# Attention, soft MoE and switch MoE in one kernel: block sums of values moved beside a pair's first scores, their copy moved to ScalarE, exponentials signalled singly

## The reference

```python
# q, k, v: (4 batches, 8 heads, 768, 64); nb = 24 blocks of 32 keys
k_sum = k.reshape(B, H, nb, block, D).max(axis=3)
v_sum = v.reshape(B, H, nb, block, D).mean(axis=3)
mask_l = np.abs(pos[:, None] - pos[None, :]) < window      # window = 16
scores_l = scale * q @ k.T
scores_s = scale * q @ k_sum.T + np.log(block)
a = softmax(concat([where(mask_l, scores_l, -1e9), scores_s]))
x = a @ concat([v, v_sum])
```

## Time and profile before

| | us |
|---|---|
| median of 3 runs (lowest, highest) | 379.94 (379.44, 381.62) |
| the profiled execution, device time | 379.92 |
| its span, first to last instruction | 378.2 |
| PE, DVE, ACT, POOL busy over the span | 326.6, 175.9, 143.6, 101.1 |
| attention stage, to the last weighted values | about 122.5 |
| granted TensorE clock, mean over the span | 0.969 of full speed |

### The profile page before, as it was taken

How to read it: one execution, slowest core, us unless ns; L and a number is a source line. 1 busy time by engine, 2 the same in 40 slices (tenths; PEclk the granted TensorE clock), 3 DMA queues, 4 the chain that set the end, 5 groups by cost and what they waited for, 6 DMA issues and landing times.

```text
span 378.2 us, 9016 instructions
## 1 busy us (share of the span) xinstructions
PE 326.6 (86%) x3272; PEld 233.9 (62%) x3273; DVE 175.9 (47%) x406; ACT 143.6 (38%) x329; POOL 101.1 (27%) x181
## 2 busy tenths in 40 slices
PE   0879879889898999969877795999999999999991
PEld 0556656667677754232325264788888888888880
DVE  2577867877885553360116596132331323213231
ACT  1476666666876422310110262123232322313221
POOL 5665675676764000000000000121211212112121
PEclk9999999999999999987998999699999999999996
DMA  7999999999999716999942900110101111010110
GB/s 306 362 425 408 414 423 415 419 419 420 410 385 406 297 50 227 383 390 405 393 156 83 364 2 0 57 47 36 55 28 55 41 42 55 28 55 34 49 56 32
DMA packets 23851, 81.64 MB, mean 216 GB/s; under 512 B 2312, under 2 KB 2312, under 8 KB 21776
## 3 DMA queue, kind: packets, MB, share of 16 engines
q1 hardware_dynamic: 20640, 73.08, 49.1%
q0 software_dynamic: 1920, 6.29, 4.4%
q10 hardware_dynamic: 1264, 1.92, 1.5%
HBM read 74.99 MB, written 6.29 MB: 215 GB/s over the span
## 4 chain that ended last, share of the span: by engine, by line
PE 57%; DMA 16%; DVE 11%; ACT 4%; POOL 4%; issue 4%; SPq 2%; ACTq 0%; DVEq 0%; POOLq 0%
PE ps L904 33%; DMA ring<-in_vt 11%; DMA ring<-in_moe_w 5%; PE ps L630 3%; POOL ring L503 3%; PE ps L643 3%; PE ps L890 3%; PE ps L600 3%; ACT work L962 2%; PE ps L787 2%; SPq L285 2%; PE ps L746 2%; DVE ps L1128 2%; PE ps L651 1%; PE ps L709 1%
## 5 line engine op out<-in xcount | busy, mean ns | idle before, releaser
L904 PE MATMUL ps<-high_w2b,hid_high 128*128 (+1 forms) x184 | 73.1, 397 | 4.1 <-DVE hid_low L1372 4.1
L904 PE MATMUL ps<-low_w2b,hid_high 128*128 (+1 forms) x184 | 72.8, 396 | 0.0
L904 PE MATMUL ps<-high_w2b,hid_low 128*128 (+1 forms) x184 | 72.5, 394 | 0.0
L962 ACT ACTIVATE work<-ps,small 128x120 f32<-128x120 f32 x192 | 53.9, 368 | 39.3 <-DVE small L1132 39.1
L556 POOL DMA_INDIRECT out_x<-work,small x24 | 23.6, 982 | 150.2 <-DVE small L1365 61.5
L1372 DVE SCALAR_TENSOR_TENSOR hid_low<-ps,hid_high 128x1024 fp32r<-128x1024 f32 x26 | 31.8, 1225 | 57.3 <-ACT hid_high L1062 57.3
L1044 ACT ACTIVATE work<-ps,small 128x512 f32<-128x512 f32 x24 | 16.5, 689 | 99.0 <-PE ps L904 99.0
L904 PEld LDWEIGHTS ps<-high_w2b,hid_high 128*128 128x128 f32 x184 | 35.3, 192 | 11.6 <-issue 4.5
L600 PE MATMUL ps<-ident,work 128*120 128x128 f32 x192 | 31.8, 289 | 10.8 <-ACT work L962 10.6
L904 PEld LDWEIGHTS ps<-high_w2b,hid_low 128*128 128x128 f32 x184 | 35.2, 191 | 7.5
L904 PEld LDWEIGHTS ps<-low_w2b,hid_high 128*128 128x128 f32 x184 | 35.3, 192 | 7.0
(11 more groups left out here) (230 smaller groups left out, 368.7 us busy)
## 6 DMA issues: line engine op xcount, KB each, us to landing
ring<-in_moe_w SPq DMA_DIRECT2D x13, 2048.0 KB, 13.4
ring<-in_qk SPq DMA_DIRECT2D x16, 1104.0 KB, 14.5
ring<-in_v SPq DMA_DIRECT2D x16, 780.0 KB, 10.1
ring<-in_moe_w SPq DMA_DIRECT2D x10, 512.0 KB, 11.3
ring<-in_vt SPq DMA_DIRECT2D x7, 384.0 KB, 8.8
comb<-in_vt SPq DMA_DIRECT2D x7, 384.0 KB, 8.2
x_or_g<-in_moe_w SPq DMA_DIRECT2D x1, 2048.0 KB, 9.0
whole_w2b<-in_moe_w SPq DMA_DIRECT2D x4, 512.0 KB, 9.0
```

Of the source, the lines that this page charges most:

```text
L904: last = pe.matmul(ps[:, 4 + u, :], hidden_part[:, u, m * P:(m + 1) * P], matrix[:, bass.ds(e * UNIT + m * DM, DM)], start=m == 0 and i == ...
L962: last = act.activation(probs[u][:, j, :], sc[u][:, j // 2, (j % 2) * KC:(j % 2 + 1) * KC], ACT.Exp, bias=negmax[u][:, j:j + 1], scale=flo ...
```

## The change

Five edits. The block sums' matmul of pair n (n of 1 and more) now stands at the head of `scores(3n)`, behind its wait for `gaps_filled`, and writes into unused columns of the score buffer. Its copy to `vsum` goes from DVE to ACT, behind the four exponentials of `exps(3n)`. Pair 0 keeps a copy on DVE, with a semaphore of its own (`first_vsum`). On POOL `fill_sums(0)` now stands ahead of `halve(1)`. Each of the four exponentials signals `exp_done`, and each of the four transposes waits for its own.

```diff
             def scores(b, s):
                 pair, g, u = s // NG, s % NG, s % 2
                 if g == 0:
                     pe.wait_ge(gaps_filled, b * NPAIR + pair + 1)
                     pe.sem_inc(pair_started, 1)
+                    if not (isinstance(b, int) and b * NPAIR + pair == 0):
+                        pe.wait_ge(vb_ready, b * NPAIR + pair)
+                        sums_by_block(block_sums[u], pair)
...
             def probs_T(b, s):
-                pe.wait_ge(exp_done, b * NSTEP + s + 1)
                 for j in range(4):
+                    pe.wait_ge(exp_done, (b * NSTEP + s) * 4 + j + 1)
                     last = pe.transpose(pt[s % 2][0:KC, j, :], probs[s % 2][:, j, :], ident[:, :])
...
             def weighted_values(b, s):
...
-                if g == 0:
-                    ahead_pair(sums_by_block, b, pair + 1, u)
...
             fill_gaps(0)
+            fill_sums(0)
             halve(1)
-            fill_sums(0)
...
                 for j in range(4):
-                    last = act.activation(probs[u][:, j, :], sc[u][:, j // 2, (j % 2) * KC:(j % 2 + 1) * KC], ACT.Exp,
-                                          bias=negmax[u][:, j:j + 1], scale=float(D) ** -0.5)
-                last.then_inc(exp_done, 1)
+                    act.activation(probs[u][:, j, :], sc[u][:, j // 2, (j % 2) * KC:(j % 2 + 1) * KC], ACT.Exp,
+                                   bias=negmax[u][:, j:j + 1], scale=float(D) ** -0.5).then_inc(exp_done, 1)
+                if s % NG == 0 and not (isinstance(b, int) and b * NSTEP + s == 0):
+                    n = b * NPAIR + s // NG
+                    act.wait_ge(vsum_done, n + 1)
+                    act.wait_ge(sums_filled, n)
+                    act.activation(vsum[3 * SLAB:4 * SLAB, 1:1 + P], block_sums[u], ACT.Copy).then_inc(vsum_ready, 1)
...
             def attended(b, s):
...
-                if g == 0:
-                    ahead_pair(copy_block_sums, b, pair + 1, u)
```

More of the change, by code:

```diff
@@ L200, in attention_soft_moe_switch_moe @@
         av = [flat[:, (6 + u) * BANK:(7 + u) * BANK] for u in range(2)]
-        block_sums = [av[u][3 * SLAB:4 * SLAB, BANK - P:BANK] for u in range(2)]
+        first_sums = av[0][3 * SLAB:4 * SLAB, BANK - P:BANK]
+        block_sums = [flat[3 * SLAB:4 * SLAB, 2 * u * BANK + BANK // 2:2 * u * BANK + BANK // 2 + P] for u in range(2)]
         disp_T = [ps[:, 2 + u, 0:S // 2] for u in range(2)]
@@ L222, in attention_soft_moe_switch_moe @@
         vT_loaded = [sem(f"vT_loaded{u}") for u in range(2)]; vb_ready = sem("vb_ready"); first_vb = sem("first_vb")
-        vsum_done = sem("vsum_done"); vsum_ready = sem("vsum_ready"); sums_filled = sem("sums_filled")
+        vsum_done = sem("vsum_done"); vsum_ready = sem("vsum_ready"); first_vsum = sem("first_vsum"); sums_filled = sem("sums_filled")
         kmax_ready = sem("kmax_ready"); gaps_filled = sem("gaps_filled"); pair_started = sem("pair_started"); top_seq = sem("top_seq")
@@ L479, in fill_sums @@
                 b, pair = n // NPAIR, n % NPAIR
-                pool.wait_ge(vsum_ready, n + 1)
+                if n:
+                    pool.wait_ge(vsum_ready, n)
+                else:
+                    pool.wait_ge(first_vsum, 1)
                 pool.wait_ge(v_loaded[pair], b * 16 + 16)
@@ L572, in _, with sums_by_block @@
             pe.wait_ge(consts_ready, 1)
+            def sums_by_block(to, pair):
+                pe.matmul(to, vb[pair % 2], ident[:, :], start=True, stop=True, tile_position=(0, 3 * SLAB),
+                          skip_group_check=True).then_inc(vsum_done, 1)
             def scores(b, s):
@@ L665, in _ @@
             scores(0, 0)
-            sums_by_block(0, 0, 0)
+            pe.wait_ge(first_vb, 1)
+            sums_by_block(first_sums, 0)
             scores(0, 1)
@@ L1141, in halve_first @@
                 dve.tensor_tensor(vb[0][:, 0:NB], t[:, 0:NB], t[:, NB:2 * NB], ALU.add).then_inc(first_vb, 1)
[L1143 to L1151, removed]
             def attended(b, s):
@@ L1183, in _ @@
             row_max(0, 0)
-            copy_block_sums(0, 0, 0)
+            dve.wait_ge(vsum_done, 1)
+            dve.tensor_copy(vsum[3 * SLAB:4 * SLAB, 1:1 + P], first_sums).then_inc(first_vsum, 1)
             row_max(0, 1)
```

## The result

| | before | after |
|---|---|---|
| median, us (runs) | 379.88 (4) | 403.56 (4) |
| lowest, highest | 379.44, 381.62 | 403.37, 404.06 |
| span of the profiled execution | 378.2 | 401.8 |
| granted clock, mean | 0.969 | 0.942 |

The ratio is 1.0619, with a 95% interval of 1.0589 to 1.0649: slower by 23.7 us. The forecast was 401.1, its range 397 to 410.

The account below looks back on a forecast made before the run. Engine-to-engine latency was taken to bound attention, with the change closing a POOL loop of 8.38 us per pair. Over 14 turns, the stage ends 21.2 us later: 379.9 + 21.2 = 401.1 us, range 397 to 410.

Parts of the forecast that it names:

- The circle: Attention: `fill_sums`, `halve`, `fill_gaps`, scores, row maximum, exponentials, ACT copy, next `fill_sums`, strictly in sequence; 8.38 us per pair.
- the turn: Attention stage, one pair, from one `fill_sums` to the next: 6.63 us before, forecast 8.38 us after.
- four exponentials until ACT starts the next instruction: 0.98: On ACT, time from the start of a step's exponentials to the start of the block sums' copy: 0.98 us.
- The sum: `fill_sums(1)` at 19.57 plus 14 x 8.38 gives `fill_sums(15)` at 136.89; stage ends 21.2 us later, total 401.1.
- The tail: Attention from step 45's row maximum to the last weighted values: three steps as before, signals taking perhaps 0.4 us off.
- The clock rival: PE pauses of about 2.0 us lower the clock in attention, 0.7 us more per low turn; 404 to 412, chance 0.24.
- its case of half the turns: Low clock in half of the 14 attention turns, each costing 0.7 us more: 405.9 us.
- The faster rival: Attention's previous chain decides, shortened by up to 0.67 of 6.63 us, DMA the floor; down to 375.2, chance 0.03.
- its point of decision: POOL's wait between `fill_gaps` and `fill_sums`: under 1.76 us would mean a faster kernel.
- the old chain: Attention before: scores, row maximum, exponentials, transposes, weighted values and back, 6.63 us per pair, losing the moved copy and matmul.
- worth up to 0.67 per pair: Gain in attention's previous chain from moving out the DVE copy and block sums' matmul, hidden by POOL's wait.
- The other edits: Attention: earlier transposes, up to about 0.5 us, covered by the wait; `fill_sums(0)` first starts pair 0 sooner, no further profit.

Follow-up runs that it names:

- keep_busy: Changed kernel with seven unused 128x128 matmuls added on PE ahead of the wait for `gaps_filled` of each pair but the first; 404.96 us.
- one_wait: Changed kernel without the ACT copy's wait for `vsum_done`; 403.79 us.
- double_copy_apart: Changed kernel with a second ACT copy of the block sums, to unused columns, ahead of the real one from pair 1 on; 407.03 us.
- sums_between: Changed kernel with POOL's order `halve(n+1)`, `fill_sums(n)`, `fill_gaps(n+1)` from pair 1 on; 380.58 us.
- copy_first: Changed kernel with the ACT copy of the block sums ahead of the four exponentials of the pair's first step; 388.94 us.
- pool_order: Changed kernel with POOL's `halve(n+1)` and `fill_gaps(n+1)` both ahead of `fill_sums(n)` from pair 1 on; 392.61 us.

## Why the prediction was right

**The circle.** Shown. All its terms but one came within 0.01 us of their rows. Taking a link out shortened the turn, adding to a link lengthened it, and opening the circle on POOL (without closing another) took back the loss, up to 0.7 us that the runs can't tell from nothing. POOL's wait doubled from 1.76 to 3.66.

**The term that was mis-sized** is "four exponentials until ACT starts the next instruction: 0.98". I took it from a copy of 120 rows behind exponentials of 128; the new copy of 32 rows starts at 1.14. Over 14 turns that is 2.2 us. The copy itself I had from two longer ones, right within 0.01. The Trainium skill, ScalarE: Activation LUTs, section What ACT_TABLE_LOAD costs, gave 1.10 and 0.29, by the estimate from it 403.2. Its sum was nearer, but its overlap of about 93 ns between all successive instructions isn't what the rows show: 117 ns between exponentials before the change and none ahead of this copy.

**The sum.** `fill_sums(15)` came at 139.40, forecast 136.89: 0.24 from the start (19.81 for 19.57), 2.3 from 14 turns of 8.54 on average. Thirteen of these were 8.51 to 8.60; the first was 8.74, at full clock, since PE answered POOL in it only after 0.33 us instead of 0.15, and no run shows why. The tail was to be 0.4 shorter than before and was 0.8 longer (136.98 to 147.23, 10.25, against 9.47). The low clock accounts for the 0.8, since the same stretch took 9.47 in `keep_busy` and in `one_wait`, at full clock. That is also the length before the change, so the 0.4 that the signals were to save wasn't there. The stages after it took 1.1 us less than before (401.8 - 147.2 = 254.6 against 255.7), which I had as no change; in the other kernels they took from 253.2 to 257.4, with other positions of the low stretches, and I did not take that apart. The row maximum of step 45 lay 2.42 ahead of `fill_sums(15)` (139.40 - 136.98) where I had 2.26, which takes 0.2 off. So 401.1 + 0.2 + 2.3 - 0.2 + 1.2 - 1.1 = 403.5. That the tail and the stages after it nearly cancel is luck, and so is the close agreement of this sum with the median: the profiled execution took 404.06, since 2.3 us lay around its span of 401.8, where the forecast had taken 1.7 as before.

**The clock rival** was half right. Once the pauses were there, the clock fell in every second turn. The section HAM oscillation of the Trainium skill's page TensorE: Matmul & The Clock Gate tells of a clock lost in each wait. The trace agrees only in part: the clock fell in half of the turns, and the waits that the section tells of are longer than the 2 us here, so I made too much of it in calling this rival the forecast by that section. The rival's condition came out much as in its case of half the turns, 405.9, but its price was wrong for where the clock fell: PE's slack of 2 us swallowed it in six of seven cases. Where a low stretch met the circle it cost 0.65 in one turn of `one_wait` and 0.5 in each of two turns of `double_copy_apart`, near the 0.7 I had given it. I had read that price from the start of the trace, where the granted clock reads 1.00; only the length of the scores, 1.01 us, speaks for the low level there, since they take as long in the rows at 0.50 after the change and 0.58 at full clock. From the second low stretch on, the pause that followed a low stretch was 0.9 to 1.0 us and the one ahead of it 1.9 to 2.0.

**The faster rival** fell for its stated reason, and its point of decision held: POOL's wait was above 1.76. But what it took as given, that the moved work leaves the old chain, is also wrong, as `sums_between` shows; my "worth up to 0.67 per pair" came to 0.07 there (turns of 6.56 for 6.63).

**The other edits.** The signals are worth about 1 us in the kernel before. In the changed kernel nothing of them shows, since no term of the circle holds them and the tail was not shorter, but no run took them out of it. `fill_sums(0)` first is worth nothing measurable.

## What to carry to other kernels

When a step moves, follow what waits for it once round, through the orders of the engines that aren't edited: if the way comes back to the step's own new predecessor, add up every link, since none of them can be hidden. An engine's wait ahead of its step (here 1.76 us on POOL) is the room that a move may use up, however idle the engine is on average. Opening one such circle can close the next, and a step that moves from one engine to another may stay on the same chain.

## What was not expected of the hardware

ACT instructions in a row overlap by 0.11 to 0.14 us from 128 rows to 128 or 120, by 0.09 from 32 to 32, and not at all from 128 to 32, from 32 to 120 or, in `copy_first`, from 32 to 128 rows.

The granted clock fell to 0.50 in the changed kernel with pauses of PE of 2 us between dense work of 6.5 us, and did not in `copy_first`, where none was over 1.3. But the length of the last pause alone doesn't settle it: in the changed kernel the clock stayed full after a pause of 2.11 us at 22.9 us and first fell after one of 1.37, and in `pool_order` and `sums_between` one stretch of about 7 us at 0.50 followed a single pause of 2.85 and 2.52.
